# An opening re-ordered: idle products, loads from two queues, and two heads' states in one tile

## The chip, the cores and the metric

One Trainium2 chip, one core of it. The metric is the device time of the core in microseconds, median of several executions. The engines are TensorE (PE in the profile, with its weight loads as PEld), VectorE (DVE), ScalarE (ACT), GpSimd (POOL) and SyncE (SP), which issues transfers; ScalarE can issue them too (ACTq).

## The reference

Three parts in float32. First a gated linear attention over 4 batches, 8 heads, 768 steps and a head dimension of 48:

```python
f = 1.0 / (1.0 + np.exp(-f_logit))
for t in range(S):
    state = f[:, :, t, :, None] * state + np.einsum('bhd,bhe->bhde', k[:, :, t], v[:, :, t])
    y[:, :, t] = np.einsum('bhd,bhde->bhe', q[:, :, t], state)
```

Its output, turned to 3072 rows of 384, goes through a mixture of four experts (384 to 1024, ReLU, 1024 to 384, weighted by normalised domain probabilities), and that through a soft mixture of eight experts with four slots each. The change touches the attention and the start of the first mixture alone.

## The kernel before

The attention works in chunks of 128 steps and in halves of a batch (384 steps, three chunks, BT = 3). A half has 8 heads. Four heads of a half are a quad (16 of them, index m), two heads are a unit (32 of them, index u = 2m, 2m+1; four units make a half, index k). The gates are used as sums of logarithms: k is multiplied by the exponential of the summed logs and q by its inverse, so that within a chunk the scores are one masked product of q and k, and between chunks a state of 48 by 48 per head is carried. A unit of a late half (`carried(u)`) takes in a state from the half before.

The order of work on every engine is one list, `STEPS`. Its first part is written by hand (`OPENING`), the rest comes from `first_stage`. Every engine walks the same list and does its own part of each step:

- `G m` exponential of the logits on ScalarE (L824) and a clamp on DVE (L1027); `L m` logarithm on ScalarE (L829) and the sums of logs on GpSimd (L595 to L601).
- `C m`, `D m` sums within a chunk on PE (L1380, L1382), growth on ScalarE (L855, L856: exponentials of the sums), and multiplication with k and q on DVE (L1047, L1049). C takes chunks 0 and 1, D chunk 2.
- `T u` turns q and k (PE L1420, L1424; copies to qT on ScalarE L860 and to kT on DVE L1058). `S u` scores (PE L1438), mask (DVE L1065) and states (DVE L1075, L1080). `P u` products of k and v (PE L1446). `Y u` outputs: masked scores by v (PE L1464) and q by the state (PE L1469), both added up in one bank of PSUM, then copied to yT (ScalarE L866).
- SP copies yT to `x_raw` (`rows_out`, L679: `x_raw<-yT`, five transfers for each two units). `X k` splits `x_raw` into two parts of reduced precision, xT high (ScalarE L887) and low (DVE L1123). It begins with `stepped(k)`, in which ScalarE and DVE each read a flag from memory and, if gates were extreme, recompute the half step by step.
- `R i` issues expert weights from ScalarE's queue (L907, L908), `W f` splits them (ScalarE L898, L899, GpSimd L626, L627). `h k.f` and `s k.f` are the hidden product (PE L1487 to L1489, relu L894, L1142) and the second product (PE L1505 to L1507) of the first expert.

The heads of a unit lie one below the other in partition windows of 64 (WIN). The states `st` and `carry` have room for both heads side by side, `[P, ..., 2, D]`: the rows of head 0 are filled only in its own columns and the rest stays zero, so that L1469 can go over all 128 rows of qT. DVE writes each head's state by itself, on 64 partitions.

Loads of f, k, q and v come in chunks of 96 KB. At the start SP issues f of quads 0 and 1, then k, q, v of quad 0, k, q, v of quad 1 and, after waits, those of quad 2. After every second unit `next_loads(u)` issues f, k and q of quad u//2 + 3; for u = 1 these (quad 3) stand between the row copies of units 1 and 2.

From unit 5 on, hidden and second products of the first expert are interleaved with the units, and after unit 31 PE does nothing but experts.

Of the kernel before, what the change touches and what calls it, by code (L numbers as in the profile page):

```python
# [9 lines left out]
ALU = mybir.AluOpType  # L10
# [3 lines left out]
P = 128  # L14
# [14 lines left out]

OPENING = (  # L30
    "G0 L0 G1 C0 D0 L1 T0 T1 S0 P0 S1 P1 C1 D1 Y0 Y1 R0 T2 T3 G2 S2 P2 S3 P3 L2 Y2 Y3 C2 D2 R2 W0 "
    "T4 S4 P4 W1 X0 h0.0 G3 Y4 h0.1 W2 s0.0 L3 R4 W3 C3"
# [3 lines left out]
SPLIT_FROM = 4  # L36
SPLITS = {5: (4,), 6: (5, 6), 7: (7,)}
# [4 lines left out]
def first_stage(f_tiles):  # L42

    steps = []
# [11 lines left out]
    for u in range(LAG, UNITS + 1):  # L56
        n = begun + 4 * (u - LAG) - sum(1 for w in SHORT if w < u)
        if u == UNITS:
            last = pieces.index(("h", HALVES - 2, f_tiles - 1))
            steps += pieces[n:last]  # L60
            steps.append(("X", HALVES - 1, None))
            steps += pieces[last:]
            break
# [14 lines left out]
        if u % PER_HALF == 0:  # L78
            steps.append(("X", u // PER_HALF - 1, None))
# [25 lines left out]
def build(nc, q, k, v, f_logit, probs, w1, w2, phi, v1, v2, out, y_slow):  # L105
# [133 lines left out]
    st = [small("st0", [P, BT - 1, 2, D]), small_at(second, "st1", [P, BT - 1, 2, D])]  # L239
    carry = small("carry", [P, PER_HALF, 2, D])  # L240
# [85 lines left out]
    with ctx:  # L326
# [153 lines left out]
        def st_count(u):  # L480

            return sum(2 * (BT - 1 if carried(w) else BT) for w in range(u))
# [21 lines left out]
        N_CONSTS, N_ZEROED = 4, 2 + 4  # L504
# [143 lines left out]

        @block.sync
        def _(sp):  # L650
            def load_f(m):
                b, late, h0 = place(m)
                for c in range(BT):
                    sp.dma_start(f_in[m % 2][:, c].rearrange("p (h d) -> p h d", d=D),
                                 f_dram[b, BT * late + c, :, h0:h0 + QH]).then_inc(f_landed[m % 2], 16)

            def load_kq(m):
                b, late, h0 = place(m)
                for c in range(BT):
                    sp.dma_start(k_in[m % 2][:, c].rearrange("p (h d) -> p h d", d=D),  # L660
                                 k_dram[b, BT * late + c, :, h0:h0 + QH]).then_inc(kq_landed[m % 2], 16)
# [19 lines left out]

            def next_loads(u):

                m = u // 2 + 3
                if m < QUADS:
                    sp.wait_ge(c_filled, 2 * (m - 1))
                    sp.wait_ge(log_summed, 2 * (m - 1))
                    load_f(m)
                    sp.wait_ge(kd_done, 2 * (m - 1))
                    sp.wait_ge(qd_done, 2 * (m - 1))  # L690
                    load_kq(m)
# [3 lines left out]
            load_f(0)  # L695
            load_f(1)
            load_kq(0)
# [118 lines left out]
        def _(act):  # L816
            a = nc.scalar

            a.preload_act_table_set("natural_log_exp_and_others")
# [58 lines left out]
            def x_high(k):  # L878
                b, late = divmod(k, 2)
                stepped(k)  # L880
# [23 lines left out]
            for kind, i, f in STEPS:  # L904
# [16 lines left out]
                elif kind == "Y":  # L921
                    outputs(i)
                elif kind == "X":
# [89 lines left out]
        def _(dve):  # L1013
# [3 lines left out]
            d.memset(carry[:], 0.0).then_inc(zeroed, 1)  # L1017
            for t in st:
                d.memset(t[:], 0.0).then_inc(zeroed, 1)
# [40 lines left out]
            def scores(u):  # L1060
# [6 lines left out]
                for c in range(BT):  # L1067
                    if c == BT - 1 and carried(u):
                        continue
                    for hh in range(2):  # L1070
                        rows = slice(WIN * hh, WIN * (hh + 1))
                        new = products_of(u, c)[rows, :]
                        into = carry[rows, r, hh, :] if c == BT - 1 else st[s][rows, c, hh, :]
                        if c == 0 and not carried(u):
                            ins = d.tensor_copy(into, new)  # L1075
                        else:
                            old = st[s][rows, c - 1, hh, :] if c else carry[rows, r, hh, :]
                            if c:
                                dve.wait_ge(st_done, st_count(u) + 2 * (c - 1) + hh + 1)
# [711 lines left out]
```

## Time and profile before

| | us |
|---|---|
| median of 3 runs | 1040.3 (1040.15 to 1040.63) |
| profiled execution | 1038.17 |
| its span | 1036.4 |
| PE busy in the span | 1001.4 (97%) |
| DVE, ACT, POOL busy | 360.1, 287.0, 121.6 |

The span is the time from the first to the last instruction of one profiled execution. A matrix product of float32 operands leaves two records on PE. Durations of PE records overlap, since products are pipelined: the pace is read from one start to the next, or from the start of one group to that of the next, not from the durations.

### The profile page before, as it was taken

The numbers are of one execution on the slowest core, as the hardware profiler recorded it, in microseconds if no ns is written. First come the engines' busy times: TensorE is split into PE (matmuls) and PEld (weight loads), VectorE is DVE, ScalarE is ACT, GpSimd is POOL, SyncE is SP. The second block draws the span as 40 slices with busy tenths as digits, with TensorE's granted clock in tenths as the row PEclk, the third lists the DMA queues.
The fourth block names the chain that finished last, engine by engine and source line by source line (L and its number), as shares of the span: only waits on it lengthen the run. The fifth ranks groups of instructions, "written<-read, shape, count | busy, mean of one in ns | idle before, by whom it ended". The sixth has DMA issues, their size and how long they took to land.

```text
span 1036.4 us, 17965 instructions
## 1 busy us (share of the span) xinstructions
PE 1001.4 (97%) x7018; PEld 948.1 (91%) x7018; DVE 360.1 (35%) x781; ACT 287.0 (28%) x603; POOL 121.6 (12%) x146
## 2 busy tenths in 40 slices
PE   6699999999999999999999999999999999999995
PEld 5588999999899999999999999999999999999842
DVE  5356456465553222222222222222222222222333
ACT  4354344334322411111123111111322222222322
POOL 2253112211200500000005000000230000000000
PEclk9999999999999999999999999999999999999996
DMA  8733433334313030000001100000030004011785
GB/s 171 168 75 77 90 65 77 73 62 95 62 25 135 6 122 1 0 0 0 0 1 52 69 0 0 0 0 0 0 122 1 2 1 183 0 61 63 243 305 183
DMA packets 131122, 67.05 MB, mean 65 GB/s; under 512 B 106864, under 2 KB 126832, under 8 KB 131056
## 3 DMA queue, kind: packets, MB, share of 16 engines
q1 hardware_dynamic: 128368, 63.03, 22.3%
q10 hardware_dynamic: 2688, 3.15, 1.0%
q8 instruction: 40, 0.66, 0.3%
q14 instruction: 26, 0.21, 0.1%
HBM read 56.72 MB, written 4.72 MB: 59 GB/s over the span
## 4 chain that ended last, share of the span: by engine, by line
PE 93%; DVE 3%; issue 2%; ACT 1%; POOL 1%; DMA 0%; ACTq 0%; SPq 0%; DVEq 0%; POOLq 0%
PE ph L1487 13%; PE po L1505 13%; PE po L1507 13%; PE po L1506 13%; PE ph L1489 13%; PE ph L1488 13%; PE pair L1438 2%; PE pc L1464 2%; PE pc L1469 1%; PE pair L1446 1%; PE po L1730 1%; PE ph L1715 1%; PE pair L1420 1%; PE pair L1424 1%; PE pair L1559 1%
## 5 line engine op out<-in xcount | busy, mean ns | idle before, releaser
L1142 DVE SCALAR_TENSOR_TENSOR h_lo<-ph,h_hi 128x384 fp32r<-128x384 f32 x256 | 142.5, 557 | 504.0 <-ACT h_hi L894 502.8
L894 ACT ACTIVATE h_hi<-ph 128x384 fp32r<-128x384 f32 x256 | 126.0, 492 | 511.6 <-PE ph L1489 511.6
L1487 PE MATMUL ph<-xT,w_hi 128*128 128x384 f32 (+1 forms) x768 | 264.2, 344 | 3.2 <-DVE xT L1123 3.2
L1505 PE MATMUL po<-w_hi,h_hi 128*128 128x384 f32 x768 | 259.9, 338 | 0.1
L1489 PE MATMUL ph<-xT,w_lo 128*128 128x384 f32 (+1 forms) x768 | 257.7, 335 | 0.0
L1488 PE MATMUL ph<-xT,w_hi 128*128 128x384 f32 (+1 forms) x768 | 257.4, 335 | 0.0
L1507 PE MATMUL po<-w_hi,h_lo 128*128 128x384 f32 x768 | 257.1, 335 | 0.0
L1506 PE MATMUL po<-w_lo,h_hi 128*128 128x384 f32 x768 | 256.8, 334 | 0.0
L1487 PEld LDWEIGHTS ph<-xT,w_hi 128*128 128x128 f32 x768 | 144.4, 188 | 11.3 <-issue 7.7
L1505 PEld LDWEIGHTS po<-w_hi,h_hi 128*128 128x128 f32 x768 | 144.2, 188 | 2.5 <-issue 1.5
L1488 PEld LDWEIGHTS ph<-xT,w_hi 128*128 128x128 f32 x768 | 144.7, 188 | 0.0
L1489 PEld LDWEIGHTS ph<-xT,w_lo 128*128 128x128 f32 x768 | 144.5, 188 | 0.0
L1506 PEld LDWEIGHTS po<-w_lo,h_hi 128*128 128x128 f32 x768 | 144.3, 188 | 0.0
L1507 PEld LDWEIGHTS po<-w_hi,h_lo 128*128 128x128 f32 x768 | 144.2, 188 | 0.0
L626 POOL TENSOR_TENSOR w_lo<-raw,w_hi 128x384 fp32r<-128x384 f32 x32 | 32.8, 1024 | 458.9 <-ACT w_hi L899 458.8
L1065 DVE TENSOR_TENSOR masked<-pair,causal 128x768 f32<-128x768 f32 x30 | 28.7, 958 | 54.0 <-PE pc L1469 42.3
L1464 PE MATMUL pc<-masked,v_in 128*48 128x128 f32 x360 | 33.4, 278 | 1.1 <-issue 1.1
L866 ACT ACTIVATE yT<-pc 128x384 f32<-128x384 f32 x30 | 14.7, 492 | 69.7 <-PE pc L1469 69.7
L627 POOL TENSOR_TENSOR w_lo<-raw,w_hi 128x384 fp32r<-128x384 f32 x32 | 33.1, 1035 | 0.0
L1438 PEld LDWEIGHTS pair<-qT,kT 64*128 64x128 f32 x360 | 22.4, 187 | 10.5 <-issue 6.0
L1163 DVE SCALAR_TENSOR_TENSOR x<-po,pn,x 128x384 f32 (+1 forms) x48 | 26.8, 612 | 13.5 <-PE po L1507 13.4
L1438 PE MATMUL pair<-qT,kT 64*128 64x128 f32 x360 | 28.2, 289 | 2.9 <-DVE kT L1058 2.8
(243 smaller groups left out, 762.6 us busy)
## 6 DMA issues: line engine op xcount, KB each, us to landing
v<-in_moe_w_dram SPq DMA_DIRECT2D x12, 1536.0 KB, 9.0
raw<-in_moe_w_dram SPq DMA_DIRECT2D x6, 1536.0 KB, 8.5
f_in<-in_f_logit_dram SPq DMA_DIRECT2D x48, 96.0 KB, 2.6
k_in<-in_k_dram SPq DMA_DIRECT2D x48, 96.0 KB, 2.6
q_in<-in_q_dram SPq DMA_DIRECT2D x48, 96.0 KB, 2.6
v_in<-in_v_dram SPq DMA_DIRECT2D x48, 96.0 KB, 2.6
out_dram<-out_sb SPq DMA_DIRECT2D x5, 768.0 KB, 5.4
x_raw<-yT SPq DMA_DIRECT2D x48, 72.0 KB, 2.2
```

Of the source, the lines that this page charges most:

```text
L626: g.tensor_tensor(w1_lo[:, f], raw_a[:, :, c], w1_hi[:, f].bitcast(F32), ALU.subtract)
L627: g.tensor_tensor(w2_lo[:, f, :], raw_b[:, f, :], w2_hi[:, f, :].bitcast(F32), ALU.subtract).then_inc(w_lo_done, 1)
L894: a.activation(h_hi[:, f % 2, :], ph[f % 2][:, 0:BLK], ACT.Relu).then_inc(h_hi_done, 1)
L1142: d.scalar_tensor_tensor(out=h_lo[:, f % 2, :], in0=ph[f % 2][:, 0:BLK], scalar=0.0, in1=h_hi[:, f % 2, :].bitcast(F32), op0=ALU.max, op1= ...
L1438: mm = t.matmul(banks[:, hh, cols], kT[s][rows, cols], qT[u % 2][rows, cols], start=True, stop=True)
L1464: mm = t.matmul(bank[WIN * hh:WIN * hh + D, cols], v_in[v_of(m)][:, c, head * D:(head + 1) * D], masked[s][:, hh, c, :], start=True, stop= ...
L1487: t.matmul(bank, wh, xh, start=(kk == 0), stop=False, skip_group_check=True)
L1488: t.matmul(bank, wh, xl, start=False, stop=False, skip_group_check=True)
L1489: mm = t.matmul(bank, wl, xh, start=False, stop=(kk == KT - 1), skip_group_check=True)
L1505: t.matmul(bank, hh, w2_hi[:, f, :], start=(f == 0), stop=False, skip_group_check=True)
L1506: t.matmul(bank, hh, w2_lo[:, f, :], start=False, stop=False, skip_group_check=True)
L1507: mm = t.matmul(bank, hl, w2_hi[:, f, :], start=False, stop=(f == FT - 1), skip_group_check=True)
```

## The change

It has five parts. Nine products into a bank that nobody reads are put ahead of PE's list. The first loads are split: ScalarE issues f's third chunk and k of quad 0, SP the rest, with q of quad 0 ahead of f of quad 1. The states of the two heads are stored one below the other, `[P, ..., D]`, DVE writes both heads in one operation on 128 partitions, and L1469 takes 64 rows of the state and of qT for each head. The loads of k and q of quad 3 move from `next_loads(1)` to `next_loads(3)`, behind the row copies of units 2 and 3. In the order of steps the reading of the flag becomes steps of its own (E on DVE, F on ScalarE), and the opening puts R0 ahead of Y1, W0 ahead of Y2, C2 ahead of Y3, D2 and W1 right behind it, and X0 ahead of R2 and S4. The memsets of `carry` and of the two `st` on DVE go away.

```diff
 OPENING = (
-    "G0 L0 G1 C0 D0 L1 T0 T1 S0 P0 S1 P1 C1 D1 Y0 Y1 R0 T2 T3 G2 S2 P2 S3 P3 L2 Y2 Y3 C2 D2 R2 W0 "
-    "T4 S4 P4 W1 X0 h0.0 G3 Y4 h0.1 W2 s0.0 L3 R4 W3 C3"
+    "G0 L0 G1 C0 D0 L1 T0 T1 S0 P0 S1 P1 C1 D1 Y0 R0 Y1 T2 T3 G2 S2 P2 S3 P3 E0 L2 W0 Y2 C2 Y3 D2 W1 F0 "
+    "T4 X0 R2 S4 P4 G3 h0.0 L3 h0.1 Y4 W2 s0.0 R4 W3 C3"
 )
+WARM = 9
...
-            steps.append(("X", u // PER_HALF - 1, None))
+            steps += [(kind, u // PER_HALF - 1, None) for kind in "EFX"]
...
-    st = [small("st0", [P, BT - 1, 2, D]), small_at(second, "st1", [P, BT - 1, 2, D])]
-    carry = small("carry", [P, PER_HALF, 2, D])
+    st = [small("st0", [P, BT - 1, D]), small_at(second, "st1", [P, BT - 1, D])]
+    carry = small("carry", [P, PER_HALF, D])
...
-            return sum(2 * (BT - 1 if carried(w) else BT) for w in range(u))
+            return sum(BT - 1 if carried(w) else BT for w in range(u))
...
+        def load_f_of(queue, m, c0, c1):
+            b, late, h0 = place(m)
+            for c in range(c0, c1):
+                queue.dma_start(f_in[m % 2][:, c].rearrange("p (h d) -> p h d", d=D),
+                                f_dram[b, BT * late + c, :, h0:h0 + QH]).then_inc(f_landed[m % 2], 16)
+
+        def load_k_of(queue, m):
+            b, late, h0 = place(m)
+            for c in range(BT):
+                queue.dma_start(k_in[m % 2][:, c].rearrange("p (h d) -> p h d", d=D),
+                                k_dram[b, BT * late + c, :, h0:h0 + QH]).then_inc(kq_landed[m % 2], 16)
...
+            def next_gates(m):
+                sp.wait_ge(c_filled, 2 * (m - 1))
+                sp.wait_ge(log_summed, 2 * (m - 1))
+                load_f(m)
+
+            def next_kq(m):
+                sp.wait_ge(kd_done, 2 * (m - 1))
+                sp.wait_ge(qd_done, 2 * (m - 1))
+                load_kq(m)
+
             def next_loads(u):
 
                 m = u // 2 + 3
+                if u == 3:
+                    next_kq(m - 1)
                 if m < QUADS:
...
+                    next_gates(m)
+                    if u > 1:
+                        next_kq(m)
...
-            load_f(0)
+            load_f_of(sp, 0, 0, BT - 1)
+            load_q(0)
             load_f(1)
-            load_kq(0)
             load_v(0)
...
+            load_f_of(act, 0, BT - 1, BT)
+            load_k_of(act, 0)
             a.preload_act_table_set("natural_log_exp_and_others")
...
-            d.memset(carry[:], 0.0).then_inc(zeroed, 1)
-            for t in st:
-                d.memset(t[:], 0.0).then_inc(zeroed, 1)
...
-                    for hh in range(2):
-                        rows = slice(WIN * hh, WIN * (hh + 1))
-                        new = products_of(u, c)[rows, :]
-                        into = carry[rows, r, hh, :] if c == BT - 1 else st[s][rows, c, hh, :]
...
+                    new = products_of(u, c)
+                    into = carry[:, r, :] if c == BT - 1 else st[s][:, c, :]
...
-                            state = st[s][:, c - 1, hh, :] if c else carry[:, r, hh, :]
-                            mm = t.matmul(bank[WIN * hh:WIN * hh + D, cols], state, qT[u % 2][:, cols],
+                            rows = slice(WIN * hh, WIN * (hh + 1))
+                            state = st[s][rows, c - 1, :] if c else carry[rows, r, :]
+                            mm = t.matmul(bank[WIN * hh:WIN * hh + D, cols], state, qT[u % 2][rows, cols],
                                           start=False, stop=True, skip_group_check=True)
...
+            for _ in range(WARM):
+                t.matmul(ph[1][:, 0:P], ident[:], causal[:], start=True, stop=True)
```

## Rows read from the trace of the kernel before

**Rows 1.** Windows: start:end, length, busy time by engine, granted clock, DMA.

```profile
0.00:40.00 40.00, 23.33 (x258) 19.84 (x258) 22.26 (x64) 16.95 (x36) 9.60 (x22) 1.00 0.84 178
...
52.50:112.00 59.50, 56.94 (x501) 52.60 (x500) 36.34 (x87) 26.34 (x63) 22.21 (x25) 1.00 0.38 75
112.00:290.00 178.00, 176.73 (x1574) 164.08 (x1573) 99.48 (x241) 68.96 (x154) 37.12 (x45) 1.00 0.38 76
```

**Rows 2.** Windows of the first loads: last two columns, DMA share and GB/s.

```profile
2.00:6.00 4.00, 0.00 (x0) 0.00 (x0) 1.19 (x3) 1.18 (x4) 0.85 (x5) 1.00 0.93 174
```

**Rows 3.** Timeline, first quad: start, length, engine, line, work, idle before and releaser.

```profile
0.81 1.28 ACT L819 ACT_TABLE_LOAD   x1 [0.81 <-PEq L1779]
0.82 3.19 SPq L654 DMA_DIRECT2D f_in<-in_f_logit_dram  x6
...
4.61 0.68 ACT L824 ACTIVATE f_in<-f_in 128x576 f32<-128x576 f32 x1 [1.42 <-DMA f_in<-in_f_logit_dram]
...
6.73 1.62 PE L1380 MATMUL ph<-f_in,causal 128*128 128x192 f32 x4 [6.73 <-ACT f_in L829]
...
9.03 0.49 ACT L855 ACTIVATE kd<-ph 128x384 f32<-128x384 f32 x1 [1.87 <-PE ph L1382]
...
11.83 0.52 PE L1420 MATMUL pair<-ident,qd 128*128 128x128 f32 x3 [1.55 <-DVE qd L1049]
...
15.67 0.43 DVE L1075 COPY st<-pair 64x48 f32<-64x48 f32 x2
...
16.03 0.92 PE L1380 MATMUL ph<-f_in,causal 128*128 128x192 f32 x4
...
17.08 0.96 DVE L1065 TENSOR_TENSOR masked<-po,causal 128x768 f32<-128x768 f32 x1
```

**Rows 4.** Timeline from T2 to the first hidden product.

```profile
21.53 0.52 PE L1420 MATMUL pair<-ident,qd 128*128 128x128 f32 x3 [0.76 <-DVE kd L1047]
...
30.15 3.84 SPq L679 DMA_DIRECT2D x_raw<-yT  x5
...
32.63 0.38 ACTq L907 DMA_DIRECT2D raw<-in_moe_w_dram  x1
...
34.66 0.52 PE L1420 MATMUL pair<-ident,qd 128*128 128x128 f32 x3 [2.08 <-DVE kd L1047]
...
38.24 1.35 ACT L887 ACTIVATE xT<-x_raw 128x384 fp32r<-128x384 f32 x3 [1.70 <-DMA x_raw<-yT]
...
40.63 0.45 PE L1487 MATMUL ph<-xT,w_hi 128*128 128x384 f32 x1 [3.16 <-DVE xT L1123]
```

**Rows 5.** Timeline behind it, to the scores of unit 5.

```profile
42.91 0.52 PE L1489 MATMUL ph<-xT,w_lo 128*128 128x384 f32 x1
...
52.19 0.49 ACT L855 ACTIVATE kd<-pc 128x384 f32<-128x384 f32 x1 [2.19 <-PE pc L1382]
...
55.08 0.94 PE L1438 MATMUL pair<-qT,kT 64*128 64x128 f32 x12 [0.70 <-DVE kT L1058]
```

**Rows 6.** Timeline of PE around unit 6, in narrow windows (tile shape behind the names).

```profile
62.64 0.33 PE L1506 MATMUL po<-w_lo,h_hi 128*128 128x384 f32 x1
62.81 0.34 PE L1507 MATMUL po<-w_hi,h_lo 128*128 128x384 f32 x1
63.08 0.94 PE L1438 MATMUL pair<-qT,kT 64*128 64x128 f32 x12
...
63.74 0.28 PE L1438 MATMUL pair<-qT,kT 64*128 64x128 f32 x2
63.95 0.26 PE L1446 MATMUL pair<-v_in,kd 128*64 128x48 f32 x2
...
65.09 0.39 PE L1464 MATMUL pc<-masked,v_in 128*48 128x128 f32 x4
65.31 0.39 PE L1469 MATMUL pc<-qT,st 128*48 128x128 f32 x4
65.63 0.45 PE L1487 MATMUL ph<-xT,w_hi 128*128 128x384 f32 x1
```

More of the change, by code:

```diff
@@ L60, in first_stage @@
             steps += pieces[n:last]
-            steps.append(("X", HALVES - 1, None))
+            steps += [(kind, HALVES - 1, None) for kind in "EFX"]
             steps += pieces[last:]
@@ L503, in build @@
         ring = [ph[0], ph[1], po[0], po[1], po[2], bT, bSY, bST]
-        N_CONSTS, N_ZEROED = 4, 2 + 4
+        N_CONSTS, N_ZEROED = 4, 3
         N_PADS = 4
@@ L651, in load_f, with load_kq, load_q @@
             def load_f(m):
-                b, late, h0 = place(m)
[L653 to L661, printed above, removed]
+                load_f_of(sp, m, 0, BT)
+            def load_kq(m):
+                load_k_of(sp, m)
+                load_q(m)
+            def load_q(m):
+                b, late, h0 = place(m)
                 for c in range(BT):
@@ L680, in rows_out @@
                                  yT[u % 2][row:row + n, :]).then_inc(rows_in[u % 2], 16)
+            def next_gates(m):
[6 more added lines that the diff above has]
+                load_kq(m)
             def next_loads(u):
                 m = u // 2 + 3
+                if u == 3:
+                    next_kq(m - 1)
                 if m < QUADS:
[L686 to L691, printed above, removed]
+                    next_gates(m)
+                    if u > 1:
+                        next_kq(m)
                 if 2 < m - 1 < QUADS:
                     load_v(m - 1)
-            load_f(0)
+            load_f_of(sp, 0, 0, BT - 1)
+            load_q(0)
             load_f(1)
-            load_kq(0)
             load_v(0)
@@ L879, in x_high @@
                 b, late = divmod(k, 2)
-                stepped(k)
                 for par in range(2):
@@ L922, in _ @@
                     outputs(i)
+                elif kind == "F":
+                    stepped(i)
                 elif kind == "X":
@@ L1069, in scores @@
                         continue
-                    for hh in range(2):
-                        rows = slice(WIN * hh, WIN * (hh + 1))
-                        new = products_of(u, c)[rows, :]
-                        into = carry[rows, r, hh, :] if c == BT - 1 else st[s][rows, c, hh, :]
[L1074 to L1079, printed above, removed]
-                            ins = d.tensor_tensor(into, new, old, ALU.add)
-                        ins.then_inc(st_done, 1)
+                    new = products_of(u, c)
+                    into = carry[:, r, :] if c == BT - 1 else st[s][:, c, :]
+                    if c == 0 and not carried(u):
+                        d.tensor_copy(into, new).then_inc(st_done, 1)
+                    else:
+                        old = st[s][:, c - 1, :] if c else carry[:, r, :]
+                        if c:
+                            dve.wait_ge(st_done, st_count(u) + c)
+                        d.tensor_tensor(into, new, old, ALU.add).then_inc(st_done, 1)
             def stepped(k):
@@ L1119, in x_low @@
                 b, late = divmod(k, 2)
-                stepped(k)
                 for kk in range(KT):
@@ L1177, in _ @@
                     scores(i)
+                elif kind == "E":
+                    stepped(i)
                 elif kind == "X":
```

## The prediction, as put on record before the change was run

> **What bounds the kernel now.** I read the shares of busy time first, then stretches of the span, then the opening in order of time. TensorE (PE) is busy for nearly all of the span, and the stretches say where it is not: it idles 16.7 us of the first 40, 2.6 us between 52.5 and 112, and 1.3 us in the 178 us after that [rows 1]. So there are two regimes. Before about 52 us the kernel is a chain through all engines and the loads; there an earlier release is worth its full time. From then on PE has work waiting, and only PE's own time counts: what DVE saves there is worth nothing, and what a PE instruction costs more is paid in full.
>
> In the opening [rows 3] the reader sees the logits of the first quad land just before ScalarE's exponential at 4.61, the first sums on PE at 6.73 at half pace (four records in 1.62 us; the same four take 0.92 at 16.03), ScalarE's growth at 9.03, the turn T0 at 11.83. Later [rows 4] come T2 at 21.53, the row copies of the third and fourth units issued by SP from 30.15, T4 at 34.66, and then a hole: ScalarE stands still for the rows until 38.24, and PE starts the first hidden product h0.0 only at 40.63, after 3.16 us of idleness. PE then runs at half pace for a few products (a record of 384 columns in 0.52 us, later in 0.33 [rows 5, 6]). S5, the first scores of the steady part, start at 55.08 [rows 5]. I use S5 as the anchor: how much earlier it starts is what the opening gains.
>
> **The change, part by part.**
>
> *Idle products.* Nine products of 128 columns are 18 records. A record of 192 columns takes about 0.32 at half pace (1.62 covers four that overlap, with the next group 1.62 later), so one of 128 takes 0.22 and all take 3.9 us: from 2.1 to about 6.0, before the gates at 6.7. They delay nothing. What they can bring is the full pace for the first sums: the ten records take some 3.5 us now and 1.9 later in the run, and the first six, which release the growth at 9.03, would be done 1.0 us earlier. Bounds: 0 to -1.0.
>
> *Two queues.* SP issues a 96 KB load every 0.53 us, six in 3.19 [rows 3]. The loads themselves run at 174 GB/s with the DMA engines 93% busy [rows 2], 0.565 us for each; with engines full it would be 0.525. So splitting the issue can bring little. But the order changes: SP now issues k and q of the first quad behind the second quad's logits (f1), and after the change q comes before f1 and ScalarE's queue puts k in as well, so f1 is the tenth to twelfth load instead of the fourth to sixth. From 2.0, twelve loads at 0.525 end at 8.3; the third ended by that count at 3.6 and was usable at 4.6, but that includes a slow start, so I add 0.7: f1 lands at 9.0. ScalarE's order is G0 L0 G1 C0: the exponential of f1 stands ahead of the first growth. It takes 0.6 of the engine, and the growth starts at 9.6 and not at 9.03. The earlier sums are wasted, and T0 moves to +0.5 (bounds -1.0, if f1 lands by 8, to +0.8). The four issues on ScalarE's queue, 2.1 us by SP's rate, stand ahead of its table load of 1.28 [rows 3], which then ends at 4.2, still ahead of the exponential at 4.6: no cost, but no margin either.
>
> The Trainium skill says the same of queues (DMA: Bandwidth & Descriptors, "Issuing engines are not separate DMA queues"): a second issuing engine saves issue time alone. By that f1 gains nothing from the second queue, and the 9.0 stands.
>
> *States below one another.* DVE's six operations on 64 partitions become three on 128, two where the state is carried. Two of them take 0.43, and six pass from 15.67 to 17.08, 0.235 each [rows 3]. A unit saves 0.7 us (0.47 carried). In the opening both units of a pair lie on the chain: masked(1) starts 0.7 earlier, the second pair's gates 1.4. PE now takes over as limit: D1's sums end at 18.3 (16.03, ten records of 0.17, and the 0.5), and Y0 and Y1 are five groups of 0.22 each and three changes of shape at 0.1 (below), 1.4, so T2 goes at 21.1 and not 21.53: -0.4. The second pair repeats it: states of unit 3 done 1.8 earlier. C2 now stands between Y2 and Y3 on PE and fills Y3's wait, and D2 follows Y3. Counting PE's items (Y2 at 25.7, C2 at 27.2, Y3 at 28.3, D2 at 29.7) and 2.3 from D2 to the turn (in the first quad, from 6.73 + 2.0 to 11.83, it is 3.1 with PE's four records at half pace, 0.65 of it), T4 starts at 32.0: -2.7.
>
> *k and q of the fourth quad behind the rows.* This takes six issues, 3.2 us, from in front of the row copies on SP; the copies then follow the outputs at once, and the raw weights R2, today issued at 32.63 in the middle of them [rows 4], come after X0. The rows of unit 3 are issued by 31.7 and land about 2 us later, at 33.7 and not at 38.2. The removed work is late next: k3, q3 are issued from 33.6 and are needed only by C3 at 42.8; R2's weights, issued at 34, are needed at 40.5. E0 and F0 move the reading of the flag out of the way. ScalarE's first xT copy starts at 33.7, DVE's first subtraction 0.5 later, and lasts about as long as a copy, 0.5 (three copies take 1.35, [rows 4]); PE has done S4 and P4 by 34.8, and h0.0 starts at 34.95: -5.7. PE has no long idle time ahead of it, so the half pace disappears, 1.3 us more. h0.0, h0.1, Y4 and s0.0 (1.55, 1.55, 1.9, 1.55) end at 41.5; C3's sums, whose GpSimd part is ordered earlier than now, release ScalarE's growth at 42.8, and S5 comes as far behind that as today (52.19 to 55.08, 2.9, [rows 5]): 45.7. Opening: **-9.4** (bounds -7 for another late landing or a slow stretch of PE, -11.5 if the start gains its 1.0).
>
> *The state products on PE.* This is the part that speaks against the change. L1469 went over all 128 rows and now goes over 64 rows, between products L1464 that keep 128. PE then changes the shape of its tile twice for every chunk. The rows show what a change of shape costs [rows 6]. Products of one shape follow each other at 0.17 (384 columns) or 0.22 for a group of four (0.11 for a pair). Entering 64*128 from 128*128 takes 0.27 (62.81 to 63.08), 0.10 too much; leaving 64*128 for 128*64 takes 0.21 after the last pair (63.74 to 63.95), 0.10 too much; from 128*48 to 128*128 the group takes 0.32, 0.10 too much. Between L1464 and L1469 there is nothing of the kind today (65.09 to 65.31, 0.22). A carried unit gets five new changes, another one three. Units 5 to 31 are 15 carried and 12 others: 75 + 36 = 111 changes of 0.098, **+10.9**. Those of units 0 to 4 are in the opening's count. Bounds: 0, if this pair of shapes is free, and 0.20 each, because the first record of 384 columns after a change also takes 0.45 and not 0.33 (65.63 and 62.64). I take 0.10: three kinds of change, rows alone, columns alone and both, all cost it.
>
> The Trainium skill (TensorEngine Tiling, "Key Properties") states that changing the tiling mode drains the engine. By it every one of the 111 changes costs; by a reading in which only a waiting engine pays, none would. The rows are on its side.
>
> *Later waits.* DVE's 0.47 to 0.7 a unit meets a PE that does not wait; of the 3.9 us of idle time after 52.5 I give it 0.2.
>
> **Sum.** The profiled execution took 1038.2 us, 1.8 of it outside the span of 1036.4; the median of the runs is 2.1 above it. 1038.2 - 9.4 + 10.9 - 0.2 = 1039.5; with the 2.1, **1041.6 us**. A measurement of this kernel can tell about 0.2%, 2.1 us, from no change.
>
> **Rivals.**
> 1. *Faster: the change between 128*48 and 64*48 is free.* For it: the two heads' products already overlap, and no row has exactly this pair. Against: the three kinds above. The 10.9 go, and the opening's own 17 changes give back about 1.1: 1029.6 us. With all 128 changes counted (111 and the opening's share, some 122), it turns faster than the bound when one costs under 0.07.
> 2. *Slower: a change also lays bare the next weight load,* 0.20 and not 0.10. For it: the longer first record of 384 columns. Against: the weights have 48 columns, not 128, and hide behind 128 columns streamed. The opening gains 1.1 less: 1038.2 - 8.3 + 22.2 - 0.2 + 2.1 = 1054. It decides from 0.11 each, where the time passes 1042.4.
> 3. *Slower: the heads' state products no longer overlap.* They would come from two row tiles and land in one bank. A group of four would take 0.43, not 0.22, in 69 groups: +14.5, so 1056. Against: they land on different partitions, as L1464's do today. The Trainium skill (TensorEngine Tiling, "Gotcha 1: PSUM Pressure") says different row tiles cannot access one bank at the same time; the rows before don't show such a pair.
> 4. *The start does what it says:* f1 lands by 8 and T0 is 1.0 earlier. 1041.6 - 1.5 = 1040.1, no change either. The reverse, PE falling back to half pace between 8.6 and 12.3, where it now idles 3.7 us as before h0.0, costs up to 1.5: 1043.
>
> **Chances.** Forecast with rival 4 inside it 0.70 (its own range 1037.5 to 1045); rival 1 0.15; rival 2 0.10; rival 3 0.05. Within the forecast some 0.07 of the 0.70 falls below 1038.2 and 0.20 above 1042.4. So faster 0.22, same 0.43, slower 0.35. The range 1033 to 1048 leaves out rival 3, most of rivals 1 and 2, and takes prices per change from 0.03 to 0.15.
>
> **What would show it.** First growth on ScalarE at 9.6, waiting on the exponential of f1; first sums at full pace; xT at about 33.7 and h0.0 near 35; S5 near 45.7. In the steady part the groups L1464 and L1469 follow each other at 0.32 and not 0.22, and the time from S5 to the last unit grows by 11 us. If that spacing stays 0.22, the prediction is wrong by ten microseconds; if S5 is before 43 or after 48, the opening is.

## The result: 0.56% slower, and where 8 us went

| | before | after |
|---|---|---|
| median (lowest to highest) | 1040.22 us (1038.31 to 1040.63, 4 runs) | 1046.28 us (1046.12 to 1046.60, 4 runs) |
| profiled execution, and its span | 1038.17, 1036.4 | 1046.12, 1044.4 |

The ratio is 1.0056, with a 95% interval of 1.004 to 1.0073: slower by 6.1 us in the medians. It lies inside the range of 1033 to 1048 and 4.7 us above the forecast of 1041.6. By the prediction's own bound (2.1 us from no change) this is slower, and the "same" that had the largest single chance did not come. In the two profiled executions the difference is 8.0 us, since that of before lies 2.1 below its median.

The page of after: DVE is lighter, as was meant (before 360.1 us in 781 instructions), and PE is still the bound.

```profile
span 1044.4 us, 17918 instructions
PE 1022.0 (98%) x7036; PEld 945.3 (91%) x7036; DVE 342.8 (33%) x698; ACT 286.8 (27%) x603; POOL 121.6 (12%) x146
```

Four anchors in the timelines say where the 8.0 us went: S5 (the first scores of unit 5), the last group of state products, the first product of the slot experts, and the end.

| anchor | before | after | change in the stretch that ends there |
|---|---|---|---|
| S5 | 55.08 | 49.38 | -5.7 |
| last state products | 323.79 | 330.60 | +12.5 |
| slot experts | 992.25 | 1000.27 | +1.2 |
| end of the span | 1036.4 | 1044.4 | 0.0 |

Windows of after: the opening as in [rows 1], a short stretch in it, S5 to the last state products, and a stretch ahead of the slot experts (start:end, length, busy time of PE, PEld, DVE, ACT and POOL, granted clock, DMA).

```profile
0.00:35.00 35.00, 28.07 (x255) 22.53 (x256) 16.91 (x43) 14.96 (x32) 8.10 (x21) 0.95 0.74 150
11.70:15.10 3.40, 3.12 (x16) 2.82 (x18) 0.98 (x3) 0.98 (x2) 0.59 (x1) 0.50 0.93 179
49.40:330.70 281.30, 279.89 (x2365) 241.33 (x2365) 135.69 (x299) 101.76 (x231) 57.79 (x68) 1.00 0.33 67
991.00:994.40 3.40, 3.40 (x17) 0.77 (x16) 1.34 (x4) 0.82 (x2) 0.82 (x1) 0.55 0.23 27
```

The same stretch of before, from S5 to the last state products:

```profile
55.00:324.00 269.00, 265.80 (x2366) 246.92 (x2366) 150.00 (x366) 102.50 (x232) 57.68 (x68) 1.00 0.34 69
```

The reader is to subtract twice. PE is busy 14.1 us longer in the same number of products, and its idle time falls from 3.2 us to 1.4, which is what the lighter DVE gives: 14.1 - 1.8 = 12.3, and 0.2 is in where the windows were cut. The last row of after goes with the +1.2: PE ran at the granted clock of 0.55, near the lower of its two levels (1.2 of 2.4 GHz), for 3.4 us. At half pace that is up to 1.7 us of time, an estimate; 1.2 is what is left of it in the difference. No product that the change touches stands there, and the experiments below show such stretches at other places.

**What PE does around unit 6.** The timeline of after, where [rows 6] are of before (the line at 74.26 is the second half of the group at 74.11, from a narrower window):

```profile
73.48 0.34 PE L1510 MATMUL ph<-xT,w_lo 128*128 128x384 f32 x1
73.75 0.42 PE L1484 MATMUL pc<-masked,v_in 128*48 128x128 f32 x4
74.11 0.42 PE L1490 MATMUL pc<-qT,carry 64*48 64x128 f32 x4
74.26 0.28 PE L1490 MATMUL pc<-qT,carry 64*48 64x128 f32 x2
74.46 0.42 PE L1484 MATMUL pc<-masked,v_in 128*48 128x128 f32 x4
74.82 0.42 PE L1490 MATMUL pc<-qT,st 64*48 64x128 f32 x4
75.17 0.43 PE L1484 MATMUL pc<-masked,v_in 128*48 128x128 f32 x4
```

The masked products (L1484, L1464 of before) and the state products (L1490, L1469 of before) follow each other from start to start at 0.355 us, and not at 0.22 as in [rows 6]: 0.135 for each change of shape. The length of a group tells much less (0.42 against 0.39), as groups overlap: the pace is read from start to start. The busy time agrees: 14.1 us over 111 changes is 0.127 each.

A group is two pairs, one product for each head. The first pair behind a change starts 0.20 behind the pair ahead of it, and the second 0.14 behind the first (74.11 to 74.26), where pairs of one shape keep 0.105. So a change costs 0.10 before the first pair and 0.035 before the second. Both parts stand in the trace of before as well, at its own changes of shape:

```profile
64.04 0.34 PE L1446 MATMUL pair<-v_in,kd 128*64 128x48 f32 x6
64.22 0.28 PE L1464 MATMUL pc<-masked,v_in 128*48 128x128 f32 x2
```

The first pair of 48 columns starts at 63.95 [rows 6], the second at 64.04, 0.09 later. Then three steps lead from 64.04 to 64.22, 0.06 each. So the second pair is 0.03 late here too. And the last of these steps, from tile 128*64 to 128*48, costs nothing: not every other tile is a change that is paid.

**The opening.** The timeline of after, where [rows 3 to 5] are of before:

```profile
2.10 4.21 PE L1536 MATMUL ph<-causal,ident 128*128 128x128 f32 x18 [2.10 <-POOL causal L571]
...
6.57 1.65 PE L1400 MATMUL ph<-f_in,causal 128*128 128x192 f32 x4 [0.26 <-ACT f_in L853]
8.02 0.62 PE L1402 MATMUL ph<-f_in,ones_f 128*128 128x192 f32 x2
8.28 0.68 ACT L848 ACTIVATE f_in<-f_in 128x576 f32<-128x576 f32 x1 [1.76 <-DMA f_in<-in_f_logit_dram]
...
8.80 0.49 PE L1402 MATMUL ph<-sums_sb,ones_f 128*128 128x192 f32 x2
8.87 0.47 ACT L879 ACTIVATE kd<-ph 128x384 f32<-128x384 f32 x1
...
10.81 0.81 POOL L601 TENSOR_TENSOR sums_sb<-f_in 128x192 f32<-128x192 f32 x1 [2.95 <-ACT f_in L853]
11.09 0.74 DVE L1071 TENSOR_TENSOR qd<-qd,q_in 128x192 f32<-128x192 f32 x1
11.98 0.87 PE L1440 MATMUL pair<-ident,qd 128*128 128x128 f32 x3 [2.70 <-DVE qd L1071]
...
19.41 0.64 PE L1484 MATMUL pc<-masked,v_in 128*48 128x128 f32 x8
...
21.04 0.64 PE L1484 MATMUL po<-masked,v_in 128*48 128x128 f32 x8
...
22.68 0.55 PE L1440 MATMUL pair<-ident,qd 128*128 128x128 f32 x3
...
30.47 0.65 PE L1484 MATMUL po<-masked,v_in 128*48 128x128 f32 x8
...
32.22 0.49 ACT L890 ACTIVATE yT<-po 128x384 f32<-128x384 f32 x1 [0.77 <-PE po L1490]
...
34.53 0.52 PE L1440 MATMUL pair<-ident,qd 128*128 128x128 f32 x3 [1.51 <-DVE kd L1069]
35.94 0.52 ACT L910 ACTIVATE xT<-x_raw 128x384 fp32r<-128x384 f32 x1 [0.36 <-SPq L765]
...
37.27 0.45 PE L1508 MATMUL ph<-xT,w_hi 128*128 128x384 f32 x1
...
44.39 0.49 PE L1400 MATMUL pc<-f_in,causal 128*128 128x192 f32 x2
...
46.41 1.16 DVE L1069 TENSOR_TENSOR kd<-kd,k_in 128x384 f32<-128x384 f32 x1 [4.63 <-ACT kd L879]
47.49 1.36 DVE L1071 TENSOR_TENSOR qd<-qd,q_in 128x384 f32<-128x384 f32 x1
49.38 0.38 PE L1458 MATMUL pair<-qT,kT 64*128 64x128 f32 x2 [1.24 <-DVE kT L1080]
```

The idle products do bring the full pace, but late: the first four sums still take 1.65 us, the next two 0.62, and only the last ones 0.49 for two records (0.85 without the idle products, shown under "What does the start bring?"). The logits of the second quad land at 8.28, ScalarE and DVE serve them first, PE idles 2.70 us, and at T0 it runs at half pace, three records in 0.87 and not 0.52; the window of 3.4 us above has the granted clock at 0.50. This is the reverse of rival 4, which the prediction had as a side case.

### The profile page after: what moved, and what is told of

The parts are those of the page before. It is cut to its first block, busy times and chain, and to the rows that moved or that the text cites. A ratio compares the mean times of both kernels' runs of the same rounds, so it can differ in the third digit from the quotient of the medians.

```text
span 1044.4 us, 17918 instructions
## 1 busy us (share of the span) xinstructions
PE 1022.0 (98%) x7036; PEld 945.3 (91%) x7036; DVE 342.8 (33%) x698; ACT 286.8 (27%) x603; POOL 121.6 (12%) x146
## 4 chain that ended last, share of the span: by engine, by line
PE 96%; DVE 2%; ACT 0%; DMA 0%; SPq 0%; issue 0%; DVEq 0%; ACTq 0%
PE ph L1508 13%; PE po L1526 13%; PE ph L1510 13%; PE po L1528 13%; PE ph L1509 13%; PE po L1527 13%; PE pc L1484 3%; PE pc L1490 3%; PE pair L1458 3%; PE pair L1466 1%; PE po L1754 1%; PE ph L1739 1%; PE pair L1440 1%; PE pair L1444 1%; PE pair L1583 1%; PE ph L1660 1%
## 5 line engine op out<-in xcount | busy, mean ns | idle before, releaser
L1484 PE MATMUL pc<-masked,v_in 128*48 128x128 f32 x360 | 34.7, 284 | 0.4 <-issue 0.4
L629 POOL TENSOR_TENSOR w_lo<-raw,w_hi 128x384 fp32r<-128x384 f32 x32 | 33.0, 1033 | 0.0
L1458 PE MATMUL pair<-qT,kT 64*128 64x128 f32 x360 | 28.3, 290 | 3.0 <-DVE kT L1080 3.0
```

What stands on the lines that cost most here:

```text
L629: g.tensor_tensor(w2_lo[:, f, :], raw_b[:, f, :], w2_hi[:, f, :].bitcast(F32), ALU.subtract).then_inc(w_lo_done, 1)
L1458: mm = t.matmul(banks[:, hh, cols], kT[s][rows, cols], qT[u % 2][rows, cols], start=True, stop=True)
L1484: mm = t.matmul(bank[WIN * hh:WIN * hh + D, cols], v_in[v_of(m)][:, c, head * D:(head + 1) * D], masked[s][:, hh, c, :], start=True, stop= ...
```

## Experiments

The kernel before was run on the same chip each time: 1040.57 us in the first four, 1040.12 in the next four, 1040.26 in the last four. "Full rows" is the kernel after with one thing taken back, the states side by side and the state products over 128 rows. Median and ratio are of all executions, the last four columns (in us) of the one that was profiled.

| run | median (range, n) | ratio [95%] | T0 | xT | S5 | S5 to last state products |
|---|---|---|---|---|---|---|
| full rows | 1030.42 (1030.12-1032.46, 4) | 0.989 [0.987, 0.991] | 12.17 | 36.58 | 49.30 | 268.8 |
| rows only | 1055.90 (1054.44-1058.99, 4) | 1.0142 [1.0113, 1.017] | 12.35 | 38.84 | 58.06 | 283.3 |
| grouped | 1033.15 (1032.59-1035.75, 4) | 0.9916 [0.9895, 0.9936] | 12.35 | 36.80 | 51.20 | 269.7 |
| no idle products | 1046.92 (1043.35-1051.10, 10) | 1.0051 [1.0032, 1.0071] | 11.76 | 35.81 | 52.18 | 281.9 |
| bridge | 1031.56 (1031.48-1033.47, 5) | 0.9919 [0.9905, 0.9933] | 12.09 | 34.92 | 47.68 | 268.3 |
| f1 first | 1032.54 (1029.29-1035.33, 5) | 0.9933 [0.9916, 0.9949] | 11.00 | 33.82 | 46.60 | 268.3 |
| one queue | 1033.32 (1030.57-1036.66, 6) | 0.9926 [0.9906, 0.9946] | 12.23 | 37.84 | 52.10 | 268.9 |
| grouped, first opens | 1034.67 (1031.84-1037.07, 6) | 0.9946 [0.9927, 0.9965] | 12.42 | 33.89 | 48.29 | 269.8 |
| both (bridge, f1 first) | 1031.71 (1030.23-1035.40, 6) | 0.9917 [0.9898, 0.9935] | 11.00 | 33.82 | 49.56 | 268.4 |
| full rows again | 1033.73 (1032.57-1038.22, 6) | 0.9946 [0.9926, 0.9967] | 12.62 | 37.28 | 49.89 | 268.3 |
| k and q in front | 1033.39 (1030.66-1036.22, 6) | 0.9932 [0.9911, 0.9953] | 12.06 | 37.62 | 51.78 | 268.8 |
| raw early | 1035.71 (1031.98-1039.98, 12) | 0.9952 [0.9937, 0.9967] | 12.54 | 36.53 | 50.70 | 268.5 |

### What does the shape of the state products cost?

**Rows only** (`e2_rows_only`): the kernel before with this edit alone.

```
-  state = st[s][:, c - 1, hh, :] if c else carry[:, r, hh, :]
-  mm = t.matmul(bank[...], state, qT[u % 2][:, cols], ...)
+  rows = slice(WIN * hh, WIN * (hh + 1))
+  state = st[s][rows, c - 1, hh, :] if c else carry[rows, r, hh, :]
+  mm = t.matmul(bank[...], state, qT[u % 2][rows, cols], ...)
```

> The kernel before with one edit: the state product of each head takes only that head's 64 rows of the state and of qT. DVE's work, the loads and the order stay. Theory, 0.135 us for each of 128 changes of shape, 111 of them where PE has no slack: 15 to 17 us slower, 1055 to 1057. Rival, only the first 0.10 counts: 11 to 13, about 1052. Rival, the loss came with the states' storage or with the order: no change, 1040.

Measured: 1055.90 us, 15.3 above before. The stretch from S5 to the last state products is 14.6 us longer than in before, with as many products (but for a few missing records) and the same work on DVE:

```profile
58.00:341.30 283.30, 280.19 (x2363) 241.05 (x2365) 150.09 (x366) 102.50 (x232) 57.65 (x68) 1.00 0.33 65
```

14.6 over 111 changes is 0.13 each. Nothing else was edited, so the slice of 64 rows is shown to be the cause of these 14.6. The other 3.0 us of its profiled execution lie ahead of S5.

**Full rows** (`e1_full_rows`): the kernel after with the reverse edit, and DVE's six operations on 64 partitions again in place of three.

> The changed kernel with its states side by side again (one head per DVE operation, the state product over all 128 rows); all else of the change stays. Theory, each change of tile shape between the masked products and the state products costs PE 0.135 us (0.20 instead of 0.10 before the first pair, 0.14 instead of 0.105 before the second): 111 of them from unit 5 on leave, 15 us, DVE gives back about 1 us in the opening: 1031 to 1033, and S5 starts between 48.5 and 50.5. Rival, the re-ordered opening is what costs the time (later loads, new waits): the time stays above 1040.

Measured: 1030.42 us, 10.2 below before; a second set of runs of the same kernel, below, gave 1033.73, 6.5 below. The order, the loads and the moved transfers, that is everything but the states, gain 0.5 to 1.1%; the states cost 15.9 us against the first set and 12.6 against the second. The timeline of its products, at the pitch of 0.22 as before:

```profile
72.94 0.39 PE L1495 MATMUL pc<-qT,carry 128*48 128x128 f32 x4
73.16 0.39 PE L1490 MATMUL pc<-masked,v_in 128*48 128x128 f32 x4
73.38 0.39 PE L1495 MATMUL pc<-qT,st 128*48 128x128 f32 x4
```

Its window answers that of after: 14.2 us less of PE's time, and 3.2 us of idle time as before, not 1.4.

```profile
49.20:318.10 268.90, 265.73 (x2365) 246.95 (x2365) 150.11 (x366) 102.33 (x231) 57.67 (x68) 1.00 0.35 71
```

**Grouped** (`e3_grouped`) and **grouped, first opens** (`e8_grouped_first`): the kernel after, with all masked products of an output ahead of all its state products, so that a unit changes shape once more than before and not three or five times. In the first, each masked product still opens its range, and part of the sums that masked products left in the bank is dropped from the output. The second opens the bank once and leaves nothing out, so the argument rests on it.

```
                 for c in range(BT):
                     ... masked products, in the second with start=(c == 0)
+                for c in range(BT):
+                    cols = slice(c * P, (c + 1) * P)
+                    inter = c > 0 or carried(u)
                     if inter:
                         ... state products
```

> The changed kernel with the products of an output in another order: the masked products of all three chunks, then the state products of all chunks, instead of chunk by chunk. The same products on the same rows, with one change of shape inside a unit instead of five or three. Theory, the price hangs on the change of shape: 84 of the 111 go, 11.3 us, and about 1 us in the opening: 1034. Rival, each product over 64 rows is dearer by itself: 1046, as the changed kernel.

> The changed kernel with an output's masked products of all chunks ahead of its state products (one change of shape inside a unit instead of five or three), and only the first chunk's masked product opens a group in the bank. Theory, 84 changes fewer from unit 5 on at 0.135 us, 11.3, and about 1 in the opening, as e3_grouped: 1033 to 1034. Rival, none of it: 1046.

Measured: 1033.15 us for the first and 1034.67 for the second, 13.1 and 11.6 below after. The states stay below one another; only the changes of shape went. The timeline and window of the second:

```profile
71.73 0.86 PE L1484 MATMUL pc<-masked,v_in 128*48 128x128 f32 x12
72.52 0.42 PE L1493 MATMUL pc<-qT,carry 64*48 64x128 f32 x4
72.77 0.60 PE L1493 MATMUL pc<-qT,st 64*48 64x128 f32 x8
```

```profile
48.20:318.10 269.90, 268.39 (x2363) 245.25 (x2365) 135.82 (x300) 101.97 (x231) 57.82 (x68) 1.00 0.35 70
```

The masked products follow each other at 0.26 a group of four (three groups from 71.73 to 72.52, with the change behind them counted in), and the 64-row ones at 0.25 (72.52 to 72.77, of which 0.035 is the second part of the change): products of 64 rows are not slow in themselves, a change is. The account closes: one change is left in each of 27 units, and PE is busy 2.7 us more than with full rows (0.10 each), while its idle time is 1.5 and not 3.2. Most of the one cancels the other: 269.8 against 268.8 us.

### What does the start bring?

**No idle products** (`e4_no_idle`): `WARM = 9` becomes `WARM = 0` in the kernel after.

> The changed kernel without the nine idle products. Theory, they bring nothing, since the first growth waits for the second quad's logits (8.28) and not for PE, and they put the full pace so early that the idle stretch before T0 is followed by half pace from 11.7 to 15.1: without them the first sums run at half pace and the turns and scores at full pace, T0 within 0.3 us of 12.0, total 1045, 1 us faster. Rival, they are worth their time: first growth and T0 later by 0.5 or more, 1047.

Measured: 1046.92 us against 1046.28, no difference. The timeline of its start has the sums at half pace, and T0 no later but at half pace too, which was not expected:

```profile
6.67 1.62 PE L1400 MATMUL ph<-f_in,causal 128*128 128x192 f32 x4 [6.67 <-ACT f_in L853]
...
9.36 0.84 PE L1402 MATMUL ph<-sums_sb,ones_f 128*128 128x192 f32 x2
11.26 0.35 DVE L1071 TENSOR_TENSOR qd<-qd,q_in 128x192 f32<-128x192 f32 x1
11.76 0.87 PE L1440 MATMUL pair<-ident,qd 128*128 128x128 f32 x3 [1.56 <-DVE qd L1071]
```

So the idle products bring the sums' end forward by 0.9 us (9.29 and 10.20). The first growth, behind f1's exponential on ScalarE, gains 0.1 of it (8.87 and 8.98), and T0 nothing: it waits for DVE, whose last multiplication took 0.74 us in after, while GpSimd was at its sums, and 0.35 here. PE is at half pace at T0 with them and without: in after it had fallen back, here it had not risen yet.

**Bridge** (`e5_bridge`), **f1 first** (`e6_f1_first`), **both** (`e9_both`) and **one queue** (`e7_one_queue`), each on top of full rows. The bridge is ten more idle products between D0 and T0, into columns of a bank that nobody reads; f1 first puts the second quad's logits ahead of the first q on SP; one queue has the first loads on SP alone, in the order of before.

```
+                if kind == "T" and i == 0:                     # bridge
+                    for _ in range(BRIDGE):
+                        t.matmul(bST[:, BLK:BLK + P], ident[:], causal[:], start=True, stop=True)
-            load_q(0)                                          # f1 first
             load_f(1)
+            load_q(0)
```

> The kernel with full-row state products (e1) and ten more idle products, in a free part of a bank, between D0's sums and T0, where PE stands still for about 3 us. Theory, it is this idle stretch and not the one ahead of the first sums that sets PE's pace in T0 to S1: with it filled the turns and scores from 12 on run at full pace, T2 starts 1 to 1.5 us earlier, total 1029 to 1030 against 1030.4. Rival, the chain there is DVE's and the pace is covered: no difference.

> e1 with the second quad's logits issued by SP ahead of the first quad's q. Theory, the first growth on ScalarE waits for these logits (its exponential starts at 8.28 and the growth at 8.87): three loads earlier they land near 7, the growth starts when the sums are done, at about 8.0 to 8.3 if PE is at full pace by then, T0 at 11.2 to 11.5 instead of 12, if q is there (needed at 9.2): 0.5 to 0.8 us less in all. Rival, q is late instead: T0 no earlier, 1030.4.

> e1 (full-row state products) with both edits of e5 and e6: ten more idle products before T0 and the second quad's logits ahead of the first quad's q. Theory, growth at 7.9 and full pace from the first sums on whatever the execution: T2 at 20.7 and less scatter, 1029 to 1030. Rival, PE's pace between executions is not in the opening's hand: median and scatter as e10.

> e1 with the first loads as in the kernel before: all on SP, f of both quads, then k and q. Theory, the DMA engines are the limit and the second queue gains at most the few tenths by which T0 now waits: the first growth at about 8.9, total within 0.5 us of 1030.4. Rival, the two queues are worth 1 us or more of the opening: 1031.5 or above.

Measured: the anchors move, the medians don't. With f1 first the exponential starts at 6.94 and the growth at 7.87, and T0 is at 11.00:

```profile
6.94 0.68 ACT L848 ACTIVATE f_in<-f_in 128x576 f32<-128x576 f32 x1 [0.41 <-DMA f_in<-in_f_logit_dram]
...
7.87 0.49 ACT L879 ACTIVATE kd<-ph 128x384 f32<-128x384 f32 x1 [0.24 <-PE ph L1408]
```

In the profiled executions of bridge and f1 first PE keeps the full pace through the opening, and S5 comes at 47.68 and 46.60, 1.6 and 2.7 ahead of full rows. But these are single executions (that of f1 first took 1029.29 us, its four others 1032.13 to 1035.33), and the medians of all four kernels, 1031.6 to 1033.3, lie within what two sets of runs of full rows themselves gave, 1030.4 and 1033.7. In the profile of both, PE ran at half pace for 6.8 us from 33.8 and again for 6.8 us from 979.3: what the start had won was gone by S5 (49.56). No gain of these edits is shown by the times, and the forecasts of 1029 to 1030 for bridge and both were missed. One queue came out at 1033.32, the mark of its rival, but full rows again came out no lower: that the second queue gains anything is not shown either.

### What does the middle of the opening bring?

**Full rows again** (`e10_full_rows_again`), **k and q in front** (`e11_kq_in_front`) and **raw early** (`e12_raw_early`), on top of full rows: the fourth quad's k and q again ahead of the row copies, and R2 again ahead of the rows.

```
-                if u == 3:                                     # k and q in front
-                    next_kq(m - 1)
                 ...
-                    if u > 1:
-                        next_kq(m)
+                    next_kq(m)
-  ... Y3 D2 W1 F0 T4 X0 R2 S4 ...                              # raw early
+  ... Y3 D2 R2 W1 F0 T4 X0 S4 ...
```

> e1 once more, as the base of this call: 1030.4, between 1029 and 1034.

> e1 with k and q of the fourth quad in front of the row copies of units 2 and 3 again. Theory of the prediction, these six issues (3.2 us) and their traffic hold the rows up: xT 2 to 4 us later than in e1 (36.6), total 1032 to 1034. Rival, the rows follow Y3, which is as late, and SP has finished by then: no difference from e10.

> e1 with the raw weights R2 issued behind D2, as before, and not behind X0. Theory, their 768 KB share the DMA engines with the rows of unit 3 and hold them up by 2 us or more: xT near 38.5, total 1032. Rival, they are in time either way and rows are small: no difference from e10.

Measured: 1033.73, 1033.39 and 1035.71 us. By the times, moving k and q alone brings nothing, and raw early is 2.0 above the first of the three, with intervals that overlap (0.9926 to 0.9967, and 0.9937 to 0.9967): unclear.

The traces tell more, if xT's start is not compared by itself. The pace of PE ahead of it differs between the executions, and so does the end of Y3's output. What the two edits do is read from that end on: the last row copy is issued behind it, lands, and lets xT start.

| run | Y3's output ends | last row copy issued | xT starts | issue behind output | xT behind issue |
|---|---|---|---|---|---|
| before | 30.97 | 33.40 | 38.24 | 2.43 | 4.84 |
| after | 32.71 | 33.35 | 35.94 | 0.64 | 2.59 |
| full rows again | 33.63 | 34.69 | 37.28 | 1.06 | 2.59 |
| k and q in front | 33.20 | 35.03 | 37.62 | 1.83 | 2.59 |
| raw early | 32.14 | 32.78 | 36.53 | 0.64 | 3.75 |

The lines for it are the two of after at 32.22 and 35.94 and these, of k and q in front (the first three) and of raw early:

```profile
32.71 0.49 ACT L887 ACTIVATE yT<-po 128x384 f32<-128x384 f32 x1 [0.37 <-PE po L1492]
35.03 0.59 SPq L691 DMA_DIRECT2D x_raw<-yT  x1
37.62 0.52 ACT L907 ACTIVATE xT<-x_raw 128x384 fp32r<-128x384 f32 x1 [1.55 <-SPq L762]
...
31.65 0.49 ACT L890 ACTIVATE yT<-po 128x384 f32<-128x384 f32 x1 [0.37 <-PE po L1495]
32.78 0.59 SPq L691 DMA_DIRECT2D x_raw<-yT  x1
36.53 1.35 ACT L910 ACTIVATE xT<-x_raw 128x384 fp32r<-128x384 f32 x3 [1.34 <-DMA x_raw<-yT]
```

In the nine other profiles of edited kernels the issue comes 0.64 to 0.68 behind the output, and in the eight of them with the raw weights behind X0 xT comes 2.58 to 2.60 behind the issue (4.81 in rows only, which has the order of before). So k and q in front do hold the last row copy up, by 1.2 us (0.8 against full rows again, which itself had one late issue), and the raw weights in front make its landing 1.2 us longer. Each edit has one profile, but the other profiles agree so closely that both effects stand out; for the medians they are too small.

## Where the prediction was right and where it was wrong

**The regimes held.** PE is the bound from S5 on, and 14 us more of PE are paid nearly in full, while DVE's saving of 14.3 us in that stretch buys 1.8.

**Cost of a change of shape: the mechanism right, the size too small.** The step that was mis-sized is "111 changes of 0.098, +10.9". It measured 14.1 in PE's busy time (0.127 each; 0.135 by the starts; 14.6 or 0.13 in the run of rows only). The count held: the runs with the same 111 give one price, and the one with 27 changes left gives 0.10. The prediction read each change from the one start behind it, the 0.10 of [rows 6], and left out the second pair, which comes 0.035 late; the trace of before shows that too (63.95 to 64.04). I put this second part down to the next weight load, as in rival 2, but no run took it apart. I had argued that 48 columns of weights hide behind 128 streamed; they nearly do. Rival 2 decided from 0.11, and its condition was met, not its price of 0.20. Rival 1 (free) fell, against 15.3 us in the run made for it. So the rule of the Trainium skill that the prediction weighed (TensorEngine Tiling, "Key Properties": a change of the tiling mode drains the engine) agrees with the trace: a change costs 0.13 us here, and every change, not those alone at which PE waits.

**Rival 3 fell.** The two heads' 64-row products, on different rows and into one bank, still overlap: a group of four in grouped, first opens takes 0.25, not 0.43. The Trainium skill's sentence on row tiles and one bank ("Gotcha 1: PSUM Pressure") would have had them apart; here they land on different partitions, and the trace does not agree with it.

**Later waits: mis-sized.** "-0.2" measured -1.8: of before's waits of PE in that stretch, the one of 1.1 us on DVE's kd went, and the one on kT fell from 1.4 to 1.1, which is 1.4 of the 1.8.

**The opening: -9.4 forecast, -5.7 in the profile,** outside its bounds of -7 to -11.5. By its own marks:

| mark | forecast | after | |
|---|---|---|---|
| first growth | 9.6 | 8.87 | f1 was there at 8.28, not 9.0 |
| T0 | 12.3 | 11.98 | first sums not at full pace; no gain by the idle products |
| T2 | 21.1 | 22.68 | D1's sums end and Y0 starts at 19.4 and not 18.3, for the half pace of 3.4 us (rival 4's reverse); Y0 and Y1 took 1.63 each (1.4 counted) |
| T4 | 32.0 | 34.53 | the same 1.6, and 0.9 more: C2's sums took 1.50 (1.1 counted), Y2 and Y3 1.6 each (1.5 and 1.4) |
| xT | 33.7 | 35.94 | Y3 late by 2.2; from Y3's first product to xT 5.5 (5.4 counted) |
| h0.0 | 34.95 | 37.27 | DVE's first subtraction as expected |
| C3's sums | 41.5 | 44.39 | 0.6 more on the way |
| S5 | 45.7 | 49.38 | 5.0 behind C3 and not 4.2: kd took 1.16 on DVE, where the same step of before took 0.56 (qd 1.36 and 1.38) |

Each mark hands its delay on: of the 3.7 us that S5 is late, 1.6 are there at T2 (1.1 by the half pace, with T0's 0.3 taken off, and 0.5 in Y0 and Y1), 0.7 more at xT, and 1.4 comes behind h0.0. Y0 to Y3 alone took 0.8 more than counted; the same price per change, set too low, is part of that.

The half pace at T0 had been put as a side case of 1.5 us. Its size was right (1.4 us from T0 to D1's end), its chance was not known. Of the thirteen profiles besides before, five have it at T0, behind an idle time of 2.52 to 3.08 us: after, full rows twice, one queue, and k and q in front; rows only and grouped fall to it 0.7 and 1.3 us later. But in f1 first PE kept the full pace behind 2.52 us, in raw early behind 3.52 and in grouped, first opens behind 3.72. So the length of the idle time before T0 alone does not decide it. [Rows 5] show another stretch in before that is not in after.

In grouped, first opens, with the states below one another and the full pace, T2 comes 8.75 us behind T0; the forecast had 8.8. With the states side by side and the full pace it is 9.70 (f1 first) and 9.71 (raw early). So the gain of the lighter states in the first two units was sized rightly, as far as single executions show.

**What the loads' part said** held, as far as the runs can tell: no gain of the second queue is shown (one queue: 1033.32, inside the scatter of full rows; T0 at 12.23 against 12.17 and 12.62). That agrees with what the Trainium skill says of issuing engines (DMA: Bandwidth & Descriptors, "Issuing engines are not separate DMA queues"); the order of the loads differs too, so it is no clean test.

The step "k and q of the fourth quad behind the rows" held as well, in its reason and in its size. From before to after, Y3's output ends 1.7 us later; the last row copy is issued 1.8 us closer behind it, now that no six issues stand ahead; and xT starts 2.25 us closer behind that issue, of which raw early shows 1.2 to be the raw weights. Together: 1.74 - 1.79 - 2.25 = -2.3, the whole of xT's gain (38.24 to 35.94). From Y3's first product to xT the forecast had 5.4 us (28.3 to 33.7), and after took 5.5 (30.47 to 35.94). What was late is Y3 itself. What gives the other 1.1 of the 2.25 was not taken apart.

**The sum.** In the profiled executions: -5.7 + 14.1 - 1.8 + 1.2 + 0.2 = +8.0, where the forecast was -9.4 + 10.9 - 0.2 = +1.3. The forecast for a profiled execution, 1039.5, is 6.6 below the 1046.12 measured. Against the medians the miss is 4.7, because before's profile lies 2.1 below its median, and after's does not: the 2.1 was an offset of one execution, not of the kernel, and that it brought the forecast nearer is luck. So is it that the lighter DVE's waits (1.6 more than forecast) took off part of what the changes (3.2) and the opening (3.7) added.

**Open:** what places the half-pace stretches. They are 3.4 to 10.2 us long in these profiles, at 11 to 22, at 33 to 47 or at 979 to 995 (in grouped also at 1017 to 1024), and nearly equal kernels have them at different places. They are worth 1.2 to some 3 us each, as much as the edits of the start, so single edits there can't be told apart by these medians.

**The best version** is full rows: 1030.42 us (0.989), again 1033.73 (0.9946), both faster than before.

## What to carry to other kernels

Before a product is cut to a smaller tile to save work on another engine, look at what stands on either side of it on TensorE: where the shapes alternate, each change is paid, and 111 of them outweighed 1% won elsewhere. If the smaller tile is wanted, put products of one shape together. Read the pace of matmuls from start to start, over the whole group behind a change and not only its first start, and price an engine that is off the path at its waits (1.8 us), not at its work (14.3 us).

## What the runs showed of the hardware

- A change between tiles 128*48 and 64*48 costs 0.13 us in either direction (0.355 against 0.22 us a group), 0.10 before the first pair of products and 0.035 before the second, and products of 64*48 among themselves run as fast as those of 128*48. A step from 128*64 to 128*48 costs nothing (0.06 from start to start, as within 128*64).
- Idle products from 2.1 to 6.3 us brought the full pace only at 8.3, and an idle stretch of 2.7 us later PE was at a granted clock of 0.50 for 3.4 us. With ten more products in that gap (bridge) the profiled execution kept 1.00, but so did f1 first without them (2.52 us idle) and raw early (3.52 us idle), so they are not shown to be the reason.
- Ahead of 8 us the column of the granted clock stands at 1.00 in every profile, also where records take twice their time; in no idle products it does so up to 15.1 us (0.85 for two records at 9.36, and 0.87 for the three of T0, which take 0.52 at full pace). In the opening the pace is to be read from the records, not from that column.
- DVE's multiplication and GpSimd's subtraction slow each other when they fall together. DVE's multiplication of 128x384 took 0.55 to 0.56 us in all 28 cases of before, and in all 28 of after, in which GpSimd was idle. Of the four cases in each trace beside GpSimd's w_lo, 0.56, 0.76, 1.35 and 1.38 us in before, and 0.77, 1.16, 1.35 and 1.36 in after; the w_lo then took 1.32 to 1.39 us three times, and 1.00 to 1.03 elsewhere. What they share, no run shows.
